# Routed rows of an eight-expert layer: transposed on TensorE through the identity, or on VectorE in blocks of 32 by 32

## The chip, the cores and the metric

The kernel runs on one core of one Trainium2 chip. The metric is the time of one execution on the device in microseconds (us), from the first instruction to the end. Three runs of the kernel before are shown, and beside them one profiled execution, whose trace is read here. Engines are named as in the profile: PE is TensorE's matmul, PEld its load of weights, DVE is VectorE, ACT is ScalarE, POOL is GpSimd, SP is SyncE; a "q" behind a name (SPq) is the engine's sequencer, where DMAs are issued.

## What is computed

Attention in a window of 64 over 4 x 8 heads of 576 x 64 gives 2304 tokens of 512 features; a gated layer (512 to 1536 and back) follows, and then a layer of eight experts, of which each token takes the two with the highest noisy logits:

```python
logits = x @ w_gate
noise_scale = np.log1p(np.exp(x @ w_noise))
noisy_logits = logits + noise_scale * noise
top2 = np.argpartition(-noisy_logits, 2, axis=1)[:, :2]
...
for e in range(E):
    for k in range(2):
        mask = top2[:, k] == e
        h = np.maximum(x[mask] @ w1[e], 0.0)
        out[mask] += top2_w[mask, k, None] * (h @ w2[e])
```

All of it is in float32. The change touches only how x[mask] comes to TensorE.

## The kernel before

**Stages.** Attention fills about the first 100 us. The gated layer runs over six chunks of 384 tokens until some 574 us. While it runs, each chunk's tokens get their experts and their places, and POOL scatters their rows (2 KB each) with indirect DMAs into `routed_rows` in DRAM, sorted by expert. The last stage is the experts' work on 43 tiles of 128 rows, in order of expert; the end gathers each token's two rows of results from `expert_rows` in DRAM, scales and adds them, and writes `out`.

**One tile t of the experts' stage.** SP loads its 128 rows of 512 floats into one of two buffers of `x_row` (a row in each partition, one DMA, L510). TensorE wants the features in the partitions, so `pe_xT` transposes the rows with four matmuls against the identity into the PSUM bank `BANK_A` (L956). DVE (`dve_xT`) writes the high part of the bank to `xT_high` (L1641) and the rest to `xT_low` (L1643): a float32 product is made of three passes of rounded parts (`PRODUCTS`). `pe_up2` (L944) makes 24 matmuls of 512 columns into banks 0 and 1, `dve_relu` (L1664) writes `relu`, `pe_hT` (L985) makes eight transposes, `dve_hT` splits them into `hT_high` and `hT_low` (L1652, L1654), `pe_down2` (L972) makes 24 more matmuls into bank 5, `dve_y` (L1671) copies that to the one buffer `y_row`, and SP stores it (L514).

**The order on each engine is written by hand**, one tile interlaced with the next. PE's turn in steady state is hT(t-1), up2(t), xT(t+1), down2(t-1). DVE's is hT(t-1), relu(t), xT(t+1), y(t-1). SP's is the load of tile t+4, which waits until the buffer's rows have been transposed (`xT_done`), and then the store of tile t, which waits for y(t). Tiles 0 to 3 are interlaced with the last chunk's routing: its logits pass over PE and ACT to DVE, which picks the experts (`dve_top2`, `dve_slots`); POOL then scatters the chunk's rows; the load of tile 3 waits until these scatters have landed; `dve_table` and `dve_table_rows` make the table of the tiles.

**Beside it** ACT loads the weights of the expert after next in 16 pieces of 512 KB as soon as a slot is free, rounds them to a high part (L1256), and POOL subtracts that for the low part (L652). POOL's end works through the chunks: it waits until the tiles that a chunk needs are stored (a wait on `y_row_out` with a count from the table), issues the gathers (L668) and adds the rows that ACT has scaled (L681).

## Time and profile before

| | us |
|---|---|
| median of 3 runs | 1123.01 |
| lowest, highest | 1121.91, 1123.09 |
| the profiled execution | 1124.06 |
| its span, from the first to the last instruction | 1122.2 |
| mean granted clock of TensorE | 0.996 of 2.4 GHz |

The span is 1.9 us under the profiled execution's own time, which is 1.05 us over the median. In the views below a time at the start of a row is counted from the span's start. A busy share is a mean over stages with different limits; what an engine waited for stands in brackets behind a row of the timeline, and the end of the program is reached by following such waits back from the last instruction. A row of the timeline joins neighbouring instructions of one line (x2, x4).

### The profile page before, as it was taken

The numbers are of one execution on the slowest core, as the hardware profiler recorded it, in microseconds if no ns is written. First come the engines' busy times: TensorE is split into PE (matmuls) and PEld (weight loads), VectorE is DVE, ScalarE is ACT, GpSimd is POOL, SyncE is SP. The second block draws the span as 40 slices with busy tenths as digits, with TensorE's granted clock in tenths as the row PEclk, the third lists the DMA queues.
The fourth block names the chain that finished last, engine by engine and source line by source line (L and its number), as shares of the span: only waits on it lengthen the run. The fifth ranks groups of instructions, "written<-read, shape, count | busy, mean of one in ns | idle before, by whom it ended". The sixth has DMA issues, their size and how long they took to land.

```text
span 1122.2 us, 20144 instructions
## 1 busy us (share of the span) xinstructions
PE 1094.8 (98%) x6285; PEld 956.3 (85%) x6286; DVE 543.2 (48%) x1166; ACT 324.2 (29%) x712; POOL 398.5 (36%) x370
## 2 busy tenths in 40 slices
PE   8989999999999999999998999999999999999995
PEld 7878999999998999999986888888888888888884
DVE  6776344353353443353446744444544544454452
ACT  7996122332431431331462011110202020200331
POOL 3557992022022021100396033150707061421585
PEclk9999999999999999999999999999999999999998
DMA  7975527013022030000356133251516142311565
GB/s 213 274 239 186 166 83 272 1 57 113 1 92 80 1 134 18 39 19 1 123 187 233 41 104 131 65 171 43 196 37 195 45 157 77 118 62 54 184 219 180
DMA packets 82731, 129.39 MB, mean 115 GB/s; under 512 B 6592, under 2 KB 38736, under 8 KB 82672
## 3 DMA queue, kind: packets, MB, share of 16 engines
q1 hardware_dynamic: 60816, 71.20, 19.4%
q10 hardware_dynamic: 16032, 38.47, 10.6%
q0 software_dynamic: 5824, 18.95, 5.0%
q8 instruction: 34, 0.56, 0.2%
q14 instruction: 25, 0.20, 0.1%
HBM read 85.87 MB, written 42.73 MB: 115 GB/s over the span
## 4 chain that ended last, share of the span: by engine, by line
PE 86%; DMA 4%; POOL 3%; issue 3%; ACT 2%; DVE 1%; POOLq 0%; SPq 0%; ACTq 0%; DVEq 0%
PE bank L781 26%; PE bank L972 18%; PE bank L944 18%; PE bank L813 13%; PE bank L985 3%; PE bank L727 2%; PE bank L956 1%; PE bank L754 1%; PE bank L737 1%; POOL token_rows_a L668 1%; PE bank L721 1%; DMA token_rows_b<-expert_rows,slots_u 1%; ACT p_sb L1109 1%; PE bank L849 1%; POOL token_rows_a L681 1%
## 5 line engine op out<-in xcount | busy, mean ns | idle before, releaser
L781 PE MATMUL bank<-x_parts,mlp_weights 128*128 128x384 f32 x1704 | 312.0, 337 | 0.0
L781 PEld LDWEIGHTS bank<-x_parts,mlp_weights 128*128 128x128 f32 x1704 | 296.8, 188 | 5.9 <-issue 0.7
L972 PE MATMUL bank<-expert_parts,hT_high 128*128 (+1 forms) x688 | 216.1, 395 | 1.4 <-DVE hT_low L1654 1.4
L944 PE MATMUL bank<-expert_parts,xT_high 128*128 (+1 forms) x688 | 215.9, 395 | 0.5 <-DVE xT_low L1643 0.5
L652 POOL TENSOR_TENSOR expert_parts<-raw_expert_a,expert_parts 128x512 fp32r<-128x512 f32 x64 | 81.4, 1301 | 259.8 <-ACT expert_parts L1256 259.7
L813 PE MATMUL bank<-mlp_weights,hidden_parts 128*128 128x512 f32 x648 | 162.1, 394 | 1.8 <-ACT y_sb L1180 1.8
L972 PEld LDWEIGHTS bank<-expert_parts,hT_high 128*128 128x128 f32 x688 | 126.1, 188 | 26.1 <-issue 1.7
L944 PEld LDWEIGHTS bank<-expert_parts,xT_high 128*128 128x128 f32 x688 | 126.0, 188 | 24.7 <-DVE xT_low L1643 0.8
L813 PEld LDWEIGHTS bank<-mlp_weights,hidden_parts 128*128 128x128 f32 x648 | 120.1, 188 | 25.2 <-ACT y_sb L1180 2.2
L972 PE MATMUL bank<-expert_parts,hT_low 128*128 (+1 forms) x344 | 134.5, 391 | 0.0
L944 PE MATMUL bank<-expert_parts,xT_low 128*128 (+1 forms) x344 | 134.4, 391 | 0.0
L619 POOL DMA_INDIRECT routed_rows<-y_sb,slot_now x36 | 35.8, 994 | 261.4 <-DVE slot_now L1482 252.3
L1256 ACT CAST expert_parts<-raw_expert_a 128x1024 fp32r<-128x1024 f32 x32 | 33.6, 1050 | 303.7 <-PE bank L972 269.3
L1671 DVE COPY y_row<-bank 128x512 f32<-128x512 f32 x43 | 29.8, 692 | 158.7 <-PE bank L972 158.1
L1409 DVE TENSOR_TENSOR hidden<-bank,sigmoid 128x384 f32<-128x384 f32 x72 | 40.1, 557 | 135.3 <-ACT sigmoid L1161 129.2
L1664 DVE TENSOR_SCALAR relu<-bank 128x512 f32<-128x512 f32 x86 | 59.3, 691 | 94.5 <-PE bank L944 94.5
L1172 ACT CAST hidden_parts<-hidden 128x384 fp32r<-128x384 f32 x72 | 37.0, 513 | 161.0 <-DVE hidden L1412 154.1
L652 POOL TENSOR_TENSOR expert_parts<-raw_expert_b,expert_parts 128x512 fp32r<-128x512 f32 x64 | 81.0, 1295 | 0.0
L1161 ACT ACTIVATE sigmoid<-bank 128x384 f32<-128x384 f32 x72 | 35.4, 492 | 149.0 <-PE bank L781 148.8
L972 PEld LDWEIGHTS bank<-expert_parts,hT_low 128*128 128x128 f32 x344 | 64.6, 188 | 13.8
L944 PEld LDWEIGHTS bank<-expert_parts,xT_low 128*128 128x128 f32 x344 | 64.6, 188 | 13.6
L1415 DVE TENSOR_TENSOR hidden_parts<-hidden,hidden_parts 128x384 fp32r<-128x384 f32 x72 | 48.5, 673 | 47.0 <-ACT hidden_parts L1172 47.0
(205 smaller groups left out, 1239.0 us busy)
## 6 DMA issues: line engine op xcount, KB each, us to landing
raw_expert_a<-in_w ACTq DMA_DIRECT2D x32, 512.0 KB, 3.6
raw_expert_b<-in_w ACTq DMA_DIRECT2D x32, 512.0 KB, 4.1
x_row<-routed_rows SPq DMA_DIRECT2D x43, 256.0 KB, 2.7
expert_rows<-y_row SPq DMA_DIRECT2D x43, 256.0 KB, 2.0
expert_rows<-zeros SPq DMA_DIRECT2D x4, 2304.0 KB, 12.7
v_sb<-in_v SPq DMA_DIRECT2D x32, 256.0 KB, 3.6
q_sb<-in_qT SPq DMA_DIRECT2D x16, 288.0 KB, 3.6
k_sb<-in_kT SPq DMA_DIRECT2D x16, 288.0 KB, 4.0
```

The lines of the kernel that those rows point to most:

```text
L619: nc.gpsimd.indirect_dma_start(out=xs_dram, out_offset=bass.IndirectOffsetOnAxis(ap=slot_now[:, t, r:r + 1], axis=0), in_=y_sb[:, t, :], i ...
L652: nc.gpsimd.tensor_tensor(ew_sb[:, slot, 2 * kind + 1, at:at + 512], raw_exp(q)[:, half * 512:half * 512 + 512], ew_sb[:, slot, 2 * kind, ...
L781: last = nc.tensor.matmul(bank[:, 0:CHUNK], w_sb[:, i, wp, at:at + P], xp[:, par, part, k, :], start=n == 0, stop=n == 3 * KB - 1)
L813: last = nc.tensor.matmul(ps[3 + t][:, 0:D], hp[:, i % 2, part, t * P:(t + 1) * P], w_sb[:, i, wp, 2 * KB * P:COLS], start=i == 0 and n == ...
L944: last = nc.tensor.matmul(ps[half][:, 0:512], (xTh, xTl)[xp][:, k, :], ew_sb[:, bass.ds(slot, 1), wp, k * F2 + half * 512:k * F2 + half * ...
L972: last = nc.tensor.matmul(ps[5][:, 0:D], (hTh, hTl)[hp][:, f, :], ew_sb[:, bass.ds(slot, 1), 2 + wp, f * D:(f + 1) * D].rearrange("p a n - ...
L985: last = nc.tensor.transpose(ps[2 + b][:, f * P:(f + 1) * P], relu[:, col:col + P], ident[:])
L1161: nc.scalar.activation(sig[:], ps[2 * i % 3][:, 0:CHUNK], ACT.Sigmoid).then_inc(sig_done, 1)
L1172: nc.scalar.copy(hp[:, i % 2, 0], h_sb[:]).then_inc(hh_done, 1)
L1409: nc.vector.tensor_tensor(h_sb[:], ps[2 * i % 3][:, 0:CHUNK], sig[:], ALU.mult).then_inc(gated, 1)
L1415: nc.vector.tensor_tensor(hp[:, i % 2, 1], h_sb[:], hp[:, i % 2, 0].bitcast(F32), ALU.subtract).then_inc(hl_done, 1)
L1664: nc.vector.tensor_scalar(relu[:, half * 512:half * 512 + 512], ps[half][:], 0.0, None, ALU.max).then_inc(relu_done, 1)
```

## The change

The four matmuls against the identity are gone from PE, for every tile, and with them `pe_xT` and the argument `between` of `pe_down2`. DVE makes one instruction in their place, a transpose of [128, 512] floats in blocks of 32 by 32, each block inside its own 32 partitions, into a new buffer `x_transposed` in SBUF; the two instructions behind it that make the high and the low part now read this buffer and no longer a PSUM bank. A block must already lie in the quarter of the partitions in which it is to end, so the load of a tile becomes four DMAs, one for each quarter s: partition 32s + r gets, for k and q from 0 to 3, the 32 floats of row 32q + r that begin at column 128k + 32s. A quarter is 64 KB, in pieces of 128 bytes. The waits move with it: DVE waits for the rows (now 64 counts a tile) and for `xT_low` of the tile before, then transposes, and waits for `up_done` as before. The loop of DVE now runs over pairs of tiles, since the buffer's number has to be known. `is_e` and `of_e` lie at another address.

```diff
-                sp.dma_start(x_row[:, buf, :], xs_dram[bass.ds(row, P), :]).then_inc(x_row_in[buf], 16)
+                rows = xs_dram[bass.ds(row, P), :].rearrange("(q r) (k s c) -> s r k q c", r=BLOCK, s=BLOCKS, c=BLOCK)
+                for s in range(BLOCKS):
+                    sp.dma_start(x_row[s * BLOCK:(s + 1) * BLOCK, buf, :].rearrange(
+                        "r (k q c) -> r k q c", k=KB, c=BLOCK), rows[s]).then_inc(x_row_in[buf], 16)
...
-        def pe_xT(pe, t, buf, before):
-
-            pe.wait_ge(x_row_in[buf], 16 * before + 16)
-            if not (isinstance(t, int) and t == 0):
-                pe.wait_ge(xTl_done, t)
-            for k in range(KB):
-                last = nc.tensor.transpose(BANK_A[:, k * P:(k + 1) * P], x_row[:, buf, k * P:(k + 1) * P], ident[:])
-            last.then_inc(xT_done, 1)
...
-                if buf is not None:
-                    pe_xT(pe, t + 1, buf, earlier)
...
-        def dve_xT(dve, t):
+        def dve_xT(dve, t, buf, earlier):
+
+            dve.wait_ge(x_row_in[buf], 16 * BLOCKS * earlier + 16 * BLOCKS)
+            if not (isinstance(t, int) and t == 0):
+                dve.wait_ge(xTl_done, t)
+            nc.vector.transpose(x_T[:].rearrange("p k t -> p (k t)"), x_row[:, buf, :]).then_inc(xT_done, 1)
+            if not (isinstance(t, int) and t == 0):
+
+                dve.wait_ge(up_done, 2 * t)
             dve.wait_ge(xT_done, t + 1)
-            if not (isinstance(t, int) and t == 0):
-
-                dve.wait_ge(up_done, 2 * t)
-            bank = BANK_A[:].rearrange("p (k t) -> p k t", k=KB)
-            nc.vector.tensor_copy(xTh[:], bank).then_inc(xTh_done, 1)
+            nc.vector.tensor_copy(xTh[:], x_T[:]).then_inc(xTh_done, 1)
             dve.wait_ge(xTh_done, t + 1)
-            nc.vector.tensor_tensor(xTl[:], bank, xTh[:].bitcast(F32), ALU.subtract).then_inc(xTl_done, 1)
+            nc.vector.tensor_tensor(xTl[:], x_T[:], xTh[:].bitcast(F32), ALU.subtract).then_inc(xTl_done, 1)
```

On PE, in the loop over the tiles, where up2 of one tile ends and down2 of the tile before begins, this stands in a row before:

```order
L944 MATMUL bank<-expert_parts,xT_high 128x512
L944 MATMUL bank<-expert_parts,xT_low 128x512
L956 MATMUL bank<-ident,x_row 128x128 x4
L961 ISA
L972 ISA
L972 MATMUL bank<-expert_parts,hT_high 128x512
```

and this now (L953 is pe_up2's line in the changed file, L969 that of pe_down2):

```order
L953 MATMUL bank<-expert_parts,xT_high 128x512
L953 MATMUL bank<-expert_parts,xT_low 128x512
L960 ISA
L969 ISA
L969 MATMUL bank<-expert_parts,hT_high 128x512
```

The four transposes are gone and nothing has taken their place.

On DVE, in the same loop, from the second half of relu(t) to the copy of y(t-1), before:

```order
L1664 TENSOR_SCALAR relu<-bank 128x512
L1636 REGISTER_ALU
L1639 ISA
L1641 CAST xT_high<-bank 128x512
L1643 TENSOR_TENSOR xT_low<-bank,xT_high 128x512
L1670 ISA
L1671 COPY y_row<-bank 128x512
```

and now:

```order
L1661 TENSOR_SCALAR relu<-bank 128x512
L1630 ISA
L1632 REGISTER_ALU
L1633 STREAM_TRANSPOSE x_transposed<-x_row 128x512
L1636 REGISTER_ALU
L1637 REGISTER_ALU
L1638 CAST xT_high<-x_transposed 128x512
L1640 TENSOR_TENSOR xT_low<-x_transposed,xT_high 128x512
L1667 ISA
L1668 COPY y_row<-bank 128x512
```

One instruction came in ahead of the two that split, and these read SBUF.

On DVE at the start of the experts' stage, around tile 1, where the last chunk's logits pass through, before:

```order
L1664 TENSOR_SCALAR relu<-bank 128x512
L1430 COPY logitsT<-bank 96x128
L1641 CAST xT_high<-bank 128x512
L1643 TENSOR_TENSOR xT_low<-bank,xT_high 128x512
L1434 COPY logits<-bank 128x48
L1652 CAST hT_high<-bank 128x512
```

and now:

```order
L1661 TENSOR_SCALAR relu<-bank 128x512
L1423 COPY logitsT<-bank 96x128
L1633 STREAM_TRANSPOSE x_transposed<-x_row 128x512
L1638 CAST xT_high<-x_transposed 128x512
L1640 TENSOR_TENSOR xT_low<-x_transposed,xT_high 128x512
L1427 COPY logits<-bank 128x48
```

The new instruction stands ahead of the copy of the logits.

## Rows read from the trace of the kernel before

**Rows 1.** The page: busy time by engine, and the chain that ended last

```profile
PE 1094.8 (98%) x6285; PEld 956.3 (85%) x6286; DVE 543.2 (48%) x1166; ACT 324.2 (29%) x712; POOL 398.5 (36%) x370
...
PE 86%; DMA 4%; POOL 3%; issue 3%; ACT 2%; DVE 1%; POOLq 0%; SPq 0%; ACTq 0%; DVEq 0%
```

**Rows 2.** Windows: us, busy PE PEld DVE ACT POOL, clock, DMA share, GB/s

```profile
797.50:809.75 12.25, 12.25 (x62) 10.23 (x61) 5.94 (x10) 2.64 (x3) 8.89 (x8) 1.00 0.64 215
809.75:822.00 12.25, 12.25 (x62) 10.23 (x61) 5.94 (x9) 0.00 (x0) 0.00 (x0) 1.00 0.12 43
```

**Rows 3.** One line, L956: duration ns min/median/max, first and last start

```profile
L956 PE MATMUL bank<-ident,x_row x172: 270/273/329, 569.7 to 1085.7; 128*128 128x128 f32 x172
```

**Rows 4.** Timeline of PE, start and us, up2 to down2, transposes between

```profile
803.30 0.40 PE L944 MATMUL bank<-expert_parts,xT_low 128*128 x1
803.53 0.60 PE L956 MATMUL bank<-ident,x_row 128*128 128x128 f32 x4
...
804.44 0.40 PE L972 MATMUL bank<-expert_parts,hT_low 128*128 x1
```

**Rows 5.** Timeline of PE, tile 2, up2 to down2, nothing between

```profile
604.98 0.39 PE L944 MATMUL bank<-expert_parts,xT_low 128*128 128x512 f32 x1
...
605.20 0.62 PE L972 MATMUL bank<-expert_parts,hT_high 128*128 128x512 f32 x2
...
605.66 0.39 PE L972 MATMUL bank<-expert_parts,hT_low 128*128 128x512 f32 x1
```

**Rows 6.** Timeline of the same steady tile: DVE, and PE's next up2

```profile
803.74 0.69 DVE L1664 TENSOR_SCALAR relu<-bank 128x512 f32<-128x512 f32 x1 [1.95 <-PE bank L944]
...
804.34 0.68 DVE L1641 CAST xT_high<-bank 128x512 fp32r<-128x512 f32 x1
...
805.06 0.69 DVE L1643 TENSOR_TENSOR xT_low<-bank,xT_high 128x512 fp32r<-128x512 f32 x1
...
810.25 0.71 PE L944 MATMUL bank<-expert_parts,xT_high 128*128 x2
```

**Rows 7.** Single lines: a DVE operation with two SBUF inputs, POOL's subtraction

```profile
L1415 DVE TENSOR_TENSOR hidden_parts<-hidden,hidden_parts x72: 557/559/1724, 110.0 to 571.2; 128x384 fp32r<-128x384 f32 x72
...
L652 POOL TENSOR_TENSOR expert_parts<-raw_expert_a,expert_parts x64: 1272/1290/1612, 557.7 to 983.9; 128x512 fp32r<-128x512 f32 x64
```

**Rows 8.** DMA from 10 to 12 us, a DMA's issue, x_row's landing

```profile
DMA packets 1355, 0.58 MB, mean 289 GB/s; under 512 B 797, under 2 KB 1231, under 8 KB 1355
...
q1 hardware_dynamic: 1355, 0.58, 102.1%
...
122.22 0.51 SPq L452 DMA_DIRECT2D raw_mlp<-in_w_val  x1
...
DMA to landing us min/median/max: 2.5/2.7/6.6
```

**Rows 9.** Timeline, start of the experts' stage: waits of PE and POOL

```profile
584.35 0.73 PE L944 MATMUL bank<-expert_parts,xT_high 128*128 128x512 f32 x2 [0.52 <-DVE xT_low L1643]
...
594.24 0.97 POOL L619 DMA_INDIRECT routed_rows<-y_sb,slot_now  x1 [5.76 <-DVE slot_now L1482]
...
598.54 0.31 PE L893 MATMUL bank<-ident,table_columns 128*1 128x43 f32 x4 [0.79 <-DVE table_columns L1573]
...
605.48 1.45 SPq L510 DMA_DIRECT2D x_row<-routed_rows  x2
...
610.35 0.66 PE L956 MATMUL bank<-ident,x_row 128*128 128x128 f32 x4 [0.90 <-DMA x_row<-routed_rows]
...
614.16 0.71 PE L944 MATMUL bank<-expert_parts,xT_high 128*128 x2
```

**Rows 10.** The end: POOL's last wait for a store, last adds, y's copies

```profile
1058.50 0.95 POOL L668 DMA_INDIRECT token_rows_a<-expert_rows,slots_u  x1 [5.01 <-DMA expert_rows<-y_row]
...
1112.20 3.70 POOL L681 TENSOR_TENSOR token_rows_b<-token_rows_b,token_rows_a 128x512 f32<-128x512 f32 x3 [3.67 <-ACT token_rows_b L1298]
...
L1671 DVE COPY y_row<-bank x5: 692/692/693, 1067.1 to 1111.3; 128x512 f32<-128x512 f32 x5
```

More of the change, by code:

```diff
@@ L21 @@
 GROUP = 3
+BLOCK = 32
+BLOCKS = P // BLOCK
 def window_start(j):
@@ L158, in attention_moe_kernel @@
     yT_last = at("yT_last", [P, CHUNK_TILES, KB, P], F32, mlp.pos)
+    under = Area(mlp.pos)
+    is_e = under.take("is_e", [P, 2 * TILES, E], F32)
+    of_e = under.take("of_e", [P, 2 * TILES, E], F32)
     xc = mlp.take("x_chunk", [P, KB, CHUNK], F32)
@@ L190, in attention_moe_kernel @@
     xTl = moe.take("xT_low", [P, KB, P], F32R)
+    x_T = moe.take("x_transposed", [P, KB, P], F32)
     relu = moe.take("relu", [P, F2], F32)
@@ L211, in attention_moe_kernel @@
     kept = moe.take("kept", [P, 2, TILES], F32)
-    is_e = moe.take("is_e", [P, 2 * TILES, E], F32)
-    of_e = moe.take("of_e", [P, 2 * TILES, E], F32)
     of_last = moe.take("of_last", [P, CHUNKS, E], F32)
@@ L900, in pe_chunk @@
                     pe_up(pe, c, i, par)
-                if last and i == FB - 1:
-                    pe_xT(pe, 0, 0, 0)
                 if not first and i == 4:
@@ L948, in pe_up2, with pe_down2 @@
                 last.then_inc(up_done, 1)
[L950 to L959 removed]
+        def pe_down2(pe, t, slot, expert):
             pe.wait_ge(expert_low, 16 * expert + 16)
@@ L968, in pe_down2 @@
                     pe.wait_ge(hTl_done, 2 * t + 1 + f // 4)
-                if between and f == FB2 - 2:
-                    between()
                 for wp, hp in PRODUCTS:
@@ L1010, in pe_experts, with tile @@
             pe_up2(pe, 2, 0, 0)
-            pe_down2(pe, 1, 0, 0, lambda: pe_xT(pe, 3, 1, 1))
+            pe_down2(pe, 1, 0, 0)
             pe.wait_ge(table_done, 1)
-            def tile(t, buf, earlier=0):
+            def tile(t):
                 now = entry(pe, t + T_SLOT, 1), entry(pe, t + T_E, E - 1)
@@ L1019, in tile @@
                 pe_up2(pe, t, *now)
-                if buf is not None:
-                    pe_xT(pe, t + 1, buf, earlier)
                 pe_down2(pe, t - 1, *before)
                 return now
-            tile(3, 0, 2)
-            tile(4, 1, 2)
+            tile(3)
+            tile(4)
             with pe.Fori(0, (ETILES - 7) // 2) as m:
-                tile(2 * m + 5, 0, m + 3)
-                tile(2 * m + 6, 1, m + 3)
-            tile(ETILES - 2, (ETILES - 1) % 2, (ETILES - 1) // 2)
-            now = tile(ETILES - 1, None)
+                tile(2 * m + 5)
+                tile(2 * m + 6)
+            tile(ETILES - 2)
+            now = tile(ETILES - 1)
             pe_hT(pe, ETILES - 1)
@@ L1692, in dve_experts @@
             dve_relu(dve, 2)
-            dve_xT(dve, 3)
+            dve_xT(dve, 3, 1, 1)
             dve_y(dve, 1)
@@ L1697, in dve_experts, with tile @@
                 dve_relu(dve, t)
-                dve_xT(dve, t + 1)
+                dve_xT(dve, t + 1, (t + 1) % 2, (t + 1) // 2)
                 extra(dve, link)
                 dve_y(dve, t - 1)
-            with dve.Fori(5, ETILES - 1) as t:
+            def tile(t, buf, earlier):
                 dve_hT(dve, t - 1)
                 dve_relu(dve, t)
-                dve_xT(dve, t + 1)
+                dve_xT(dve, t + 1, buf, earlier)
                 dve_y(dve, t - 1)
+            with dve.Fori(0, (ETILES - 7) // 2) as m:
+                tile(2 * m + 5, 0, m + 3)
+                tile(2 * m + 6, 1, m + 3)
+            tile(ETILES - 2, (ETILES - 1) % 2, (ETILES - 1) // 2)
             t = ETILES - 1
```

11 lines of the change are left out of this document (4 added, 7 removed).

## The prediction

> **What bounds the kernel now.** I read the page first: PE is busy 98% of the span, and the chain that ended last runs over PE for 86% of it [rows 1]. The windows say what that means in the stage that changes: two neighbouring tiles take 12.25 us each with PE busy for all of it, one of them while an expert's weights arrive (POOL busy 8.89 us, DMA share 0.64), one with POOL idle (DMA share 0.12) [rows 2]. So in steady state a tile costs what PE's instructions cost, whatever stands beside it, and DVE is busy for 5.94 of 12.25 us. Then I read the two ends of the stage. At its start PE waits for others three times: 0.52 for xT_low of tile 1, 0.79 for the table, 0.90 for the rows of tile 3 [rows 9]. At its end the last thing that waits for a tile is POOL, at 1058.50, for a store of y; five copies of y follow it, the last at 1111.3, and nothing waits for them: the 43 tiles are numbered 0 to 42, so the store waited for is that of tile 37 [rows 10]. From there to the end of the span, 63.7 us, gathers and adds of POOL set the time (its last adds start at 1112.20, behind ACT and a gather). What PE gains after tile 37 is therefore worth nothing.
>
> **What leaves PE.** 172 transposes, four for each of 43 tiles [rows 3]. Each row says 273 ns, but PE's instructions overlap, so I take the pitch. With transposes, the third matmul of down2 starts 804.44 - 803.30 = 1.14 us after the last one of up2 [rows 4]; in tile 2, where nothing stands between, it starts 605.66 - 604.98 = 0.68 us after it [rows 5]. A tile's transposes cost 0.46 us. An upper bound is 0.60, the merged row of the four; a lower one, if the loads of weights behind them hide less than I think, 0.40.
>
> **How many count.** PE runs xT(t+1) ahead of down2(t-1), so ahead of y(37) stand the transposes up to tile 39. Tiles 0 to 4 belong to the start, which is worked out below. Tiles 5 to 39 are 35: 35 x 0.46 = 16.1 us, all on the path. Tiles 40 to 42 come too late.
>
> **What DVE gets.** One transpose of 128 x 512. No row has one. The nearest are the DVE operations of the same shape, 0.68 to 0.69 us [rows 6]; below, 0.35, if it ran at two elements a cycle; above, twice, 1.4. I take 0.69, since it moves as many elements. The cast and the subtraction now read SBUF; I take 0.68 and 0.69 for them as before. In the steady tile DVE ends its last relu and starts the cast at 804.34; the chain now is transpose, cast, subtraction at a pitch of 0.72 [rows 6], so xT_low is ready at about 806.5 and not at 805.75. PE wants it for the next up2 at 810.25 [rows 6], and 0.46 earlier with the change: 809.79. From 804.34 that leaves 5.45 us for a chain of 2.1. What hides the new instruction is down2 of the tile before; it is hidden until it takes 4.0 us. Behind it on DVE wait y(t-1) and hT, whose inputs come only with the end of down2, shortly ahead of that next up2. DVE's load rises to about 6.6 of 11.8 us. Cost: nothing.
>
> **POOL and DVE on SBUF.** The subtraction had one input in SBUF and now has two. The row of such an operation, at 384 columns, has a median of 559 ns and a maximum of 1724, and POOL's subtraction takes 1290 ns [rows 7]: an operation of DVE can lose about 1.2 us where POOL works. In a burst of weights the chain would then take up to 2.1 + 1.2 for the subtraction, and 1.2 more if the cast is hit as well, 4.5 us in all, still under 5.45. It is hidden in steady state; it counts at the start and at the end, where these chains lie open. The Trainium skill states the rule behind it (SBUF — State Buffer, Who interferes with whom): VectorE with two inputs in SBUF, or in a 2-port mode, and GpSimd exclude each other from a shared pair of ports for a whole instruction. The long maximum in [rows 7] fits it; by the rule a cast from SBUF would be struck too, which no row here shows.
>
> **The load.** One DMA becomes four, and 128 packets of 2 KB become 2048 of 128 bytes, 128 on each of 16 engines. From 10 to 12 us the queues were full and passed 1355 packets of 428 bytes on average, 797 of them under 512 bytes, in 2 us x 16 x 1.02 = 32.7 us of engines' time: 24 ns a packet [rows 8]. The small ones cost at most that; so a tile's load costs up to 128 x 24 = 3.1 us on each engine, where now it is some 0.7 (half of 0.12 x 12.25, [rows 2]). The share in a burst goes from 0.64 to at most 0.85: not full. In time: a row with a three-level pattern takes SP 0.51 us to issue [rows 8], so four take 2 us instead of 0.34, and the landing, 2.5 to 6.6 us [rows 8], grows by up to 2.4. The load of a tile is issued some 23 us ahead of its use (two tiles), so about 9 us are hidden with 14 to spare. Behind the loads on SP and in its queue waits the store of y, which has to land within a tile (11.8 us) since y_row is one buffer; SP issues the load behind the transpose, at about 805 in this tile, and the store only behind down2 and y's copy, after 809, so that is covered as well. The Trainium skill warns here (DMA: Bandwidth & Descriptors, Specifications): under 512 bytes a transfer leaves line rate, with a read-modify-write. By that rule alone the load might be several times dearer than by its bytes; the rows above already hold that price, and the sum is made from them.
>
> **The start.** Here DVE and the load are on the path. Tile 0: DVE comes to it out of the last chunk's work at the same time as before; the chain ends 0.7 later while PE comes 0.46 earlier; I count no gain. Tile 1: PE waits already 0.52 for xT_low, and the copy of the logits, on which experts, scatter and table hang, stands behind this chain [rows 9]. It gets 0.72 longer, and POOL is at work there: +0.5 to +3, I take +0.9. Tile 2: the same chain stands ahead of the table for which PE waits 0.79 [rows 9]: +0.7 more, but that delay ends in PE's later wait. Tile 3: its load is issued at 605.48 when the scatter has landed; the scatter began at 594.24 behind DVE's slots [rows 9], so it moves by the 0.9. From 606.4: the issue of the fourth piece 1.6 us later, landing after 4.9 as before (605.48 to 610.35) plus 0.5, so about 613.4; then DVE's chain of 2.1 and 0.7 for POOL: up2 of tile 3 at 616.2, and not at 614.16 [rows 9]. That is +2.0; behind it the transposes of tile 4 are gone, -0.46. The start costs **1.6 us**, with ends at 0 and 7 (every chain hit by POOL, the load at its slowest landing in a full queue).
>
> **The end.** POOL's chain of 63.7 us stays. Three tiles' chains on DVE meet it: 0 to 4 us; I take 0.5.
>
> **Sum.** 16.1 - 1.6 - 0.5 = 14.0 us less. The profiled execution would have a span of 1122.2 - 14.0 = 1108.2 and a time of 1110.1; the median stands 1.05 below it: **1109.0**. The bounds: 35 x 0.40 = 14.0, less 7 and less 1, and 35 x 0.60 = 21 with a start at 1: 1117 and 1103. That both ends of all terms meet is unlikely.
>
> **Rivals.**
> 1. POOL and DVE block each other more than I take. Speaks for it: the maximum of [rows 7]; against it: the median there. Each open chain then loses both waits: the start 3.5, the end 4: 16.1 - 7.5 = 8.6 less, **1114.4**. This is also where the rule of the Trainium skill on the shared ports leads.
> 2. The small packets are slow beside the weights' packets, not enough to bound a tile, but tile 3 and the store behind tile 4's load come late at the start, by 6 to 10 us (the queue is full there: the slowest landing, 6.6 us, was in this stretch). 16.1 - 10 = 6 less, **1117**.
> 3. Slower: DVE's transpose is dear. The mechanism is the chain from relu to xT_low ahead of the next up2; it decides from 4.0 us for the instruction. At 5.5, eight times the row of its shape, the chain would be 1.5 us too long: 35 x (1.5 - 0.46) = +36, **1161**. Against it: every operation of this shape takes 0.7.
> 4. Slower: the load bounds the tile. It decides from 11.8 us a load, 92 ns a packet. At 18 us, a tile costs 18 and not 12.25: 34 x 5.75 = +195, **1320**. Against it: the 24 ns of [rows 8].
> 5. The change does not do what it says: PE's gain is taken back by a wait that I do not see (a landing that comes only with the fourth quarter, hT late behind a blocked DVE), and the time stays: **1123**.
>
> **How the numbers follow.** The forecast has a chance of 0.66, rival 1 0.15, rival 2 0.08, rivals 3 and 4 0.07 together, rival 5 0.04. The range holds the forecast and rival 1: 1104 to 1115.5, 0.81. A measurement of this kernel can tell about 0.2% from no change, 2.2 us. Faster by more: 0.66 + 0.15 + 0.08 = 0.89; within: 0.04; slower: 0.07.
>
> **What would show it.** Right, if in the changed kernel's trace the steady tiles are 11.8 us apart with PE busy throughout, if the transpose takes 0.7 us, if PE's wait ahead of up2 of tile 3 is 1 to 3 us, and if POOL still waits last for the store of tile 37, at about 1044, with the end 64 us behind. Wrong, if PE waits for xT_low or hT_low in steady tiles, if the loads land later than 12 us after their issue, if DVE or POOL operations of 1.5 us and more are frequent on the open chains, or if after the last wait for a store POOL's chain has grown.

## The result and the profile after

| | before | after |
|---|---|---|
| median of 4 runs, us | 1122.53 | 1110.66 |
| lowest, highest | 1121.91, 1123.09 | 1109.55, 1111.26 |
| ratio, 95% interval | | 0.9893 (0.9876 to 0.991) |
| the profiled execution | 1124.06 | 1109.55 |
| its span | 1122.2 | 1107.7 |

The forecast was 1109.0, in a range from 1104 to 1115.5, with a span of 1108.2. The page of the changed kernel begins and goes on thus (engines with busy time, share and instructions, a queue with its packets, the chain that ended last; before: [rows 1]):

```profile
PE 1076.5 (97%) x6113; PEld 940.3 (85%) x6114; DVE 587.5 (53%) x1209; ACT 324.2 (29%) x712; POOL 404.6 (37%) x370
...
q1 hardware_dynamic: 145440, 71.20, 22.9%
...
PE 87%; POOL 4%; issue 3%; DMA 2%; DVE 2%; ACT 1%; SPq 0%; POOLq 0%; ACTq 0%; DVEq 0%
```

PE has 172 instructions fewer and is 18.3 us less busy, DVE has 43 more and is 44.3 us more busy. PE still carries the chain. Two neighbouring tiles of the steady state, windows with the columns of [rows 2], the second one beside an expert's weights:

```profile
833.20:845.00 11.80, 11.80 (x58) 9.86 (x57) 6.39 (x10) 2.45 (x3) 3.60 (x3) 1.00 0.36 89
845.00:856.78 11.78, 11.78 (x57) 9.82 (x56) 8.30 (x10) 4.93 (x5) 11.78 (x10) 1.00 0.82 233
```

PE is busy for every microsecond of both, so a tile costs 11.79 where it cost 12.25. DVE's three instructions per tile, grouped over all 43 tiles (ns min/median/max):

```profile
L1633 DVE STREAM_TRANSPOSE x_transposed<-x_row x43: 697/701/712, 570.8 to 1071.2; 128x512 f32<-128x512 f32 x43
...
L1638 DVE CAST xT_high<-x_transposed x43: 426/428/1511, 571.5 to 1072.0; 128x512 fp32r<-128x512 f32 x43
L1640 DVE TENSOR_TENSOR xT_low<-x_transposed,xT_high x43: 691/693/1672, 572.4 to 1072.4; 128x512 fp32r<-128x512 f32 x43
```

The start of the stage, the timeline of PE, DVE and POOL (in brackets the wait before a row):

```profile
585.88 0.73 PE L953 MATMUL bank<-expert_parts,xT_high 128*128 128x512 f32 x2 [2.11 <-DVE xT_low L1640]
...
594.21 0.97 POOL L630 DMA_INDIRECT routed_rows<-y_sb,slot_now  x1 [5.99 <-DVE slot_now L1475]
...
612.00 0.71 DVE L1633 STREAM_TRANSPOSE x_transposed<-x_row 128x512 f32<-128x512 f32 x1 [5.42 <-DMA x_row<-routed_rows]
612.82 1.51 DVE L1638 CAST xT_high<-x_transposed 128x512 fp32r<-128x512 f32 x1
614.37 0.69 DVE L1640 TENSOR_TENSOR xT_low<-x_transposed,xT_high 128x512 fp32r<-128x512 f32 x1
...
615.41 1.21 PE L953 MATMUL bank<-expert_parts,xT_high 128*128 x2 [3.25 <-DVE xT_low L1640]
```

And the window from 612 to 620 us; its clock of 0.79 is a mixture of TensorE's two levels, 2.4 and 1.2 GHz, and PE had stood idle for 3.25 us before its row at 615.41:

```profile
612.00:620.00 8.00, 4.75 (x16) 3.72 (x15) 5.16 (x7) 0.00 (x0) 2.04 (x2) 0.79 0.77 212
```

The end, from the timeline of POOL and from the chain that ended last (start, us, what):

```profile
1045.66 0.95 POOL L679 DMA_INDIRECT token_rows_a<-expert_rows,slots_u  x1 [4.65 <-DMA expert_rows<-y_row]
```

```profile
1040.73 0.70 DVE y_row L1668
1041.60 3.30 DMA expert_rows<-y_row
...
1081.83 4.09 DMA token_rows_b<-expert_rows,slots_u
```

**Where the 14.5 us of span are.** I cut both traces at the same four events. In the last column stands what the prediction's terms say for the piece.

| piece | before | after | difference | forecast |
|---|---|---|---|---|
| first up2 to the copy of y(0) | 24.12 | 24.78 | +0.66 | |
| y(0) to y(4) | 52.06 | 52.77 | +0.71 | see below |
| y(4) to y(37), 33 tiles | 404.36 | 389.06 | -15.30 | -0.46 a tile |
| y(37) to POOL's last wait for a store | 3.68 | 4.93 | +1.25 | 0 |
| from there to the end | 63.7 | 62.0 | -1.66 | +0.5 |

The five pieces add to -14.3, and the first up2 itself came 0.16 us earlier: -14.5 in all. (Of 35 tiles' transposes, two fall into the first two pieces. The copy of y(37) came 14.1 us earlier; against 35 x 0.463 = 16.2 the start therefore lost 2.1, where the forecast had 1.6.)

### The profile page after: what moved, and what is told of

It is laid out like the page before. It is cut to its first block, busy times and chain, and to the rows that moved or that the text cites. A ratio compares the mean times of both kernels' runs of the same rounds, so it can differ in the third digit from the quotient of the medians.

```text
span 1107.7 us, 20151 instructions
## 1 busy us (share of the span) xinstructions
PE 1076.5 (97%) x6113; PEld 940.3 (85%) x6114; DVE 587.5 (53%) x1209; ACT 324.2 (29%) x712; POOL 404.6 (37%) x370
## 4 chain that ended last, share of the span: by engine, by line
PE 87%; POOL 4%; issue 3%; DMA 2%; DVE 2%; ACT 1%; SPq 0%; POOLq 0%; ACTq 0%; DVEq 0%
PE bank L792 26%; PE bank L953 18%; PE bank L969 18%; PE bank L824 13%; PE bank L982 3%; PE bank L738 3%; PE bank L765 2%; POOL token_rows_a L679 1%; PE bank L748 1%; PE bank L732 1%; PE bank L860 1%; DMA token_rows_b<-expert_rows,slots_u 1%; POOL token_rows_a L692 1%; ACT p_sb L1102 1%; PE bank L871 1%
## 5 line engine op out<-in xcount | busy, mean ns | idle before, releaser
L953 PE MATMUL bank<-expert_parts,xT_high 128*128 (+1 forms) x688 | 217.2, 397 | 6.2 <-DVE xT_low L1640 5.4
L969 PE MATMUL bank<-expert_parts,hT_high 128*128 (+1 forms) x688 | 212.0, 389 | 1.5 <-DVE hT_low L1651 1.5
L953 PEld LDWEIGHTS bank<-expert_parts,xT_high 128*128 128x128 f32 x688 | 126.6, 189 | 31.4 <-issue 4.7
L969 PEld LDWEIGHTS bank<-expert_parts,hT_high 128*128 128x128 f32 x688 | 129.0, 188 | 28.3 <-issue 1.7
L953 PE MATMUL bank<-expert_parts,xT_low 128*128 (+1 forms) x344 | 134.8, 392 | 0.0
L969 PE MATMUL bank<-expert_parts,hT_low 128*128 (+1 forms) x344 | 134.1, 390 | 0.0
L663 POOL TENSOR_TENSOR expert_parts<-raw_expert_b,expert_parts 128x512 fp32r<-128x512 f32 x64 | 86.3, 1381 | 0.6 <-ACT expert_parts L1249 0.6
L953 PEld LDWEIGHTS bank<-expert_parts,xT_low 128*128 128x128 f32 x344 | 64.8, 188 | 14.0
L969 PEld LDWEIGHTS bank<-expert_parts,hT_low 128*128 128x128 f32 x344 | 64.6, 188 | 13.4
```

Source lines behind the costliest of these rows:

```text
L663: nc.gpsimd.tensor_tensor(ew_sb[:, slot, 2 * kind + 1, at:at + 512], raw_exp(q)[:, half * 512:half * 512 + 512], ew_sb[:, slot, 2 * kind, ...
L953: last = nc.tensor.matmul(ps[half][:, 0:512], (xTh, xTl)[xp][:, k, :], ew_sb[:, bass.ds(slot, 1), wp, k * F2 + half * 512:k * F2 + half * ...
L969: last = nc.tensor.matmul(ps[5][:, 0:D], (hTh, hTl)[hp][:, f, :], ew_sb[:, bass.ds(slot, 1), 2 + wp, f * D:(f + 1) * D].rearrange("p a n - ...
```

## Experiments

The profile left two theories on the start open. **The load**: the rows come late because of the four DMAs with 128-byte pieces. **DVE and POOL**: the three operations on SBUF are held beside POOL's subtractions. A third suspect is TensorE's clock after a wait. All kernels were timed against the kernel before on the same chip; the runs lie on four chips, and before had medians of 1121.19 (the first four runs below), 1122.48 (the next four), 1124.04 (the three with PSUM) and 1123.0 (the last). The stages ahead end at slightly different moments (the first up2 between 571.9 and 577.4 us), so I compare distances:

| kernel | ratio (95%) | first up2 to y(0) | y(0) to y(4) |
|---|---|---|---|
| before | 1 | 24.12 | 52.06 |
| changed, first profile | 0.9893 (0.9876, 0.991) | 24.78 | 52.77 |
| changed, again | 0.9918 (0.9905, 0.9931) | 26.12 | 53.03 |
| plain load | 0.9906 (0.9891, 0.9922) | 26.10 | 53.13 |
| blocked load, PE transposes | 1.005 (1.0032, 1.0068) | 23.37 | 57.25 |
| PE for tiles 0 to 3 | 0.9859 (0.9839, 0.9878) | 23.38 | 49.79 |
| filled wait | 0.9894 (0.9869, 0.9918) | 26.15 | 51.44 |
| transpose into PSUM | 0.987 (0.9853, 0.9886) | 25.29 | 51.96 |
| plain load, into PSUM | 0.9827 (0.9811, 0.9844) | 24.39 | 48.06 |
| PE for tile 3 alone, others into PSUM | 0.9858 (0.9841, 0.9875) | 24.87 | 48.76 |

**1. The changed kernel again**, as the measure for the runs beside it.

> The changed kernel once more, beside the three runs that take parts of it, on their chip. Theory (A): the gain is 0.46 us a tile for tiles 5 to 39, less what the start of the experts' stage loses (about 2.3 us until down2 of tile 2, by the first profile). Expected: 11 to 13 us faster than before, ratio 0.989, y's copies 11.78 us apart, PE's wait ahead of up2 of tile 3 near 3.2 us. Rival (B): part of what was seen was the luck of one profile (the end 1.7 us shorter, a store 1.3 us later); then these two places differ in this profile while the time stays.

Median 1112.12 (1111.59 to 1112.36, 6 runs). It lost more of the start than the first profile: the clock was 0.93 from 575 to 600 us (first profile: 1.00) and the first up2 to y(0) took 1.3 us more. So the fall of the clock behind the first wait, 2.1 us long in both, comes in some executions or on some chips and not in others. Its price went on: the scatter began 21.41 us after the first up2, in the first profile 20.09.

**2. The plain load with DVE's transpose.**

```diff
-                rows = xs_dram[bass.ds(row, P), :].rearrange("(q r) (k s c) -> s r k q c", r=BLOCK, s=BLOCKS, c=BLOCK)
-                for s in range(BLOCKS):
-                    sp.dma_start(x_row[s * BLOCK:(s + 1) * BLOCK, buf, :].rearrange(
-                        "r (k q c) -> r k q c", k=KB, c=BLOCK), rows[s]).then_inc(x_row_in[buf], 16)
+                sp.dma_start(x_row[:, buf, :], xs_dram[bass.ds(row, P), :]).then_inc(x_row_in[buf], 16)
```

> The changed kernel with one plain DMA of 2 KB rows a tile in place of the four in pieces of 128 bytes; DVE's transpose stays. The rows are then laid out wrongly, so the experts work on permuted values, in the same shapes and with the same routing. Theory (A), the load costs only at tile 3, where it is waited for: rows there 1.5 us earlier, PE's wait ahead of up2 of tile 3 about 1.7 us and not 3.2, steady tiles still 11.78 apart; 1.5 to 3 us faster than the changed kernel. Rival (B), the small packets also slow weights, stores or gathers all along: steady tiles or the end get shorter as well, and it is 4 us or more faster. Rival (C), the start's loss is DVE's chain alone: no change.

1111.23 (1109.72 to 1111.58, 5 runs), 0.9 us under the changed kernel on the same chip; PE's wait ahead of up2(3) is still 3.34. Read at that point, it seemed that the load costs nothing. The timeline of DVE and POOL says otherwise:

```profile
609.85 0.71 DVE L1630 STREAM_TRANSPOSE x_transposed<-x_row 128x512 f32<-128x512 f32 x1 [0.34 <-DMA x_row<-routed_rows]
610.67 6.61 DVE L1635 CAST xT_high<-x_transposed 128x512 fp32r<-128x512 f32 x1
617.31 0.69 DVE L1637 TENSOR_TENSOR xT_low<-x_transposed,xT_high 128x512 fp32r<-128x512 f32 x1
```

```profile
607.02 5.03 POOL L660 TENSOR_TENSOR expert_parts<-raw_expert_a,expert_parts 128x512 fp32r<-128x512 f32 x4
612.01 4.97 POOL L660 TENSOR_TENSOR expert_parts<-raw_expert_b,expert_parts 128x512 fp32r<-128x512 f32 x4
```

The rows stand 4.4 us earlier than in the run before it (609.85 against 614.25), and then a cast of 0.43 us takes 6.61: it ends at 617.28, just after POOL's run of subtractions, which ends at 616.98. In the repeated changed kernel the cast ended at 616.65 behind a POOL that ended at 616.37, in the first profile at 614.33 behind 614.04. In these two, though, no more than the last two subtractions of POOL's run were left. So in run 2 the end of POOL's run, and not the landing, set the moment. Runs 9 and 10 test what the load would save if the cast were not held.

**3. The blocked load alone**, with TensorE's transposes as before.

```diff
-            pe.wait_ge(x_row_in[buf], 16 * before + 16)
+            pe.wait_ge(x_row_in[buf], 16 * BLOCKS * before + 16 * BLOCKS)
```

(and the four DMAs of the change.)

> The kernel before with the load in four parts of 128-byte pieces, and TensorE's transposes kept; the rows are laid out wrongly here too, so the experts work on permuted values. Theory (A): the load alone costs 1.5 to 3 us at tile 3 (landing later, store of y behind it) and nothing else: 1123.5 to 1126 us, steady tiles 12.25 apart. Rival (B), the packets hurt all along: over 1128 us. Rival (C): no change at all, 1122.5.

1128.01 (1122.15 to 1131.13, 9 runs): 5.6 us slower than before by the ratio, with an interval from 3.6 to 7.6. Steady tiles stay 12.25 us apart. What its profiled execution (1130.03) lost between the first up2 and the end lies at tile 3: y(0) to y(4) is 5.2 us longer. PE's wait there, and the window around it:

```profile
614.82 1.12 PE L962 MATMUL bank<-ident,x_row 128*128 128x128 f32 x4 [4.60 <-DMA x_row<-routed_rows]
```

```profile
612.00:620.00 8.00, 5.18 (x19) 4.46 (x20) 2.62 (x4) 0.00 (x0) 2.81 (x3) 0.60 0.81 216
```

The wait was 0.90 before [rows 9], so 3.7 are the load's. The rest I put down to the clock: four transposes take 1.12 where they took 0.66. In the steady state the load is free, as forecast; at the start it is not. Theory (A) had the place right and the size too low (1.5 to 3 us).

**4. TensorE transposes tiles 0 to 3 (with plain loads), DVE the rest.**

```diff
+                if isinstance(t, int) and t < 4:
+                    sp.dma_start(x_row[:, buf, :], xs_dram[bass.ds(row, P), :]).then_inc(x_row_in[buf], 16)
+                    return
...
+            pe_xT(pe, 2, 0, 1)
             pe_down2(pe, 0, 0, 0)
```

> Tiles 0 to 3 as before (plain load, transposes on TensorE, split out of PSUM), tiles 4 to 42 as in the changed kernel. Theory (A): the open chains at the start are then those of before, up2 of tile 3 starts near 614.2, the full clock holds there, and 35 or 36 x 0.46 remain: about 2.3 to 2.7 us faster than the changed kernel, near 1108 us, ratio to before 0.987. Rival (B): the loss moves to tile 4, whose blocked load is issued at the same place, and the store of y behind it: less than 1 us faster than the changed kernel.

1104.56 (1103.51 to 1106.96, 4 runs): 7.6 us under the changed kernel on the same chip, three times what I had expected. Both pieces of the start are shorter than those of the changed kernel, by 2.7 and 3.2 us, the clock is 1.00 in all windows of the start, and PE waits 0.52 at up2(1), as before the change, and not at all at up2(3). That is 6.0 us; another 1.9 is that its first up2 came earlier, at 573.18 and not at 575.11, and that is 1.1 earlier than in the kernel before (574.28), which does the same work up to there; so I count it as the execution's. The costs of the start add up: a wait, the clock behind it, the later store.

**5. The wait ahead of up2(3) filled** with 28 transposes of the identity.

```diff
+                if isinstance(t, int) and t == 3:
+                    fill(28, BANK_A)
                 pe_up2(pe, t, *now)
```

> The changed kernel with 28 transposes of the identity, into a bank that nothing reads, between hT(2) and up2 of tile 3, where PE idled 3.25 us and its clock then read 0.79 of full over 612 to 620 us. Theory (A): the idle time lowers the granted clock, and up2 of tile 3 took 6.9 us and not 5.6 for that; filled, the clock stays at 1.00 and up2(3) takes 5.6: 1.3 us faster than the changed kernel. Rival (B): the slow matmuls come from something else (the port contention, late weights): they stay slow, and the time is unchanged.

1111.36 (1109.0 to 1113.22, 4 runs). PE's window from 612 to 620 us:

```profile
612.00:620.00 8.00, 7.81 (x54) 6.91 (x53) 3.28 (x3) 1.26 (x2) 5.96 (x5) 1.00 0.99 284
```

The same window of the repeated changed kernel:

```profile
612.00:620.00 8.00, 4.76 (x23) 3.77 (x22) 5.05 (x7) 1.06 (x1) 4.37 (x4) 0.91 0.98 267
```

The clock stays at 1.00 where it was 0.91, and from 620 to 632 us it is 1.00 where it was 0.92. In both kernels up2(3) begins 16.5 us after the copy of y(0), so its operands came no sooner, and yet y(0) to y(4) takes 51.44 and not 53.03. So the idle time is what brings the clock down, and the clock alone is worth 1.6 us there. The medians do not settle it: the two ratios differ by 0.0024, and their intervals overlap.

**6 and 7. DVE's work lengthened**, by three and by six more transposes a tile from tile 6 on, each waiting for the last.

```diff
+            if not (isinstance(t, int) and t < 6):
+                for i in range(3):
+                    nc.vector.transpose(x_T[:].rearrange("p k t -> p (k t)"), x_row[:, buf, :]).then_inc(more, 1)
+                    dve.wait_ge(more, 3 * t + (i + 1 - 6 * 3))
```

> The changed kernel with three more DVE transposes (same data, same target) ahead of the one of each tile from tile 6 on: 2.3 us more on the chain from relu to xT_low. Theory (A): the chain has 3.5 us of cover behind down2 (xT_low ready at 660.4, up2 at 663.9 in the changed kernel's trace), so steady tiles stay 11.78 us apart and the time stays within 1 us. Rival (B): DVE is nearer to being the bound than its waits say (hT behind y, or GpSimd's port): tiles get longer, up to 34 x 2.3 = 78 us.

> The same with six more, 4.6 us. Theory (A): that is 1.1 us beyond the cover; tiles from 6 on are 12.8 to 13.0 us apart and PE waits for xT_low about 1.1 us in each; 34 tiles make +37 to +42 us on the changed kernel, 1148 to 1152 us, somewhat more if PE's clock falls in the waits. Rival (B): the cover is given by hT, not by xT_low: then PE's waits stand ahead of down2 instead. Rival (C): the cover is larger, and nothing changes.

Three more: 1119.27 (1116.63 to 1132.97, 10 runs), ratio 0.9985 (0.9956, 1.0014). I had expected it within 1 us of the changed kernel; that failed: against before it is 0.15% faster, where the repeated changed kernel was 0.82%, so about 7.5 us are lost. Most tiles stay 11.8 us apart, but two behind tile 4 take 12.2 and 12.7, and every tenth or so takes 13.04, where the chain stands beside POOL (5.1 us between y(4) and y(37)). Another 2.8 us come behind y(37); 1.1 of them because SP issues its store, behind four loads, 2.0 us after the copy began and not 0.9. A tile in which the chain meets POOL:

```profile
732.60 2.19 DVE L1636 STREAM_TRANSPOSE x_transposed<-x_row 128x512 f32<-128x512 f32 x3
734.83 0.71 DVE L1638 STREAM_TRANSPOSE x_transposed<-x_row 128x512 f32<-128x512 f32 x1
735.57 1.60 DVE L1643 CAST xT_high<-x_transposed 128x512 fp32r<-128x512 f32 x1
737.21 1.65 DVE L1645 TENSOR_TENSOR xT_low<-x_transposed,xT_high 128x512 fp32r<-128x512 f32 x1
```

```profile
739.20 0.72 PE L954 MATMUL bank<-expert_parts,xT_high 128*128 x2 [0.93 <-DVE xT_low L1645]
```

From 732.60 to 738.86 are 6.26 us, and PE waits 0.93: the cover is 5.3 us, where the prediction had 5.45. The transposes themselves keep their 0.71 us beside POOL; cast and subtraction are held by 1.2 and 1.0.

Six more: 1177.9 (1176.31 to 1184.65, 6 runs), ratio 1.0489 (1.0467, 1.051). A quiet tile takes 13.09, 1.3 us too long. Seven transposes, cast and subtraction take about 6.4 us, 1.0 more than the cover, and PE waits that long ahead of up2; what adds the other 0.3 is open. I had expected 1148 to 1152; the rest comes from tiles of 14.4 to 15 us in each burst of weights, from one of 20.8, in which the cast was held for as long as POOL worked, and from the clock (mean 0.97 between 660 and 1020 us):

```profile
951.63 8.11 DVE L1643 CAST xT_high<-x_transposed 128x512 fp32r<-128x512 f32 x1
```

```profile
949.58 4.98 POOL L664 TENSOR_TENSOR expert_parts<-raw_expert_a,expert_parts 128x512 fp32r<-128x512 f32 x4
954.53 4.92 POOL L664 TENSOR_TENSOR expert_parts<-raw_expert_b,expert_parts 128x512 fp32r<-128x512 f32 x4
```

That is the exception. In the same run five casts met runs of POOL's subtractions at nearly the same point, 0.80 to 0.84 us into one of them, and took 0.72 to 0.77; the one above began 0.78 us into one. One of the five:

```profile
679.85 0.77 DVE L1643 CAST xT_high<-x_transposed 128x512 fp32r<-128x512 f32 x1
```

**8. PE's work put back in one place**: 48 transposes of the identity between up2(4) and down2(3).

```diff
                 pe_up2(pe, t, *now)
+                if isinstance(t, int) and t == 4:
+                    fill(48, BANK_A)
```

> The changed kernel with 48 transposes of the identity (5.1 us of TensorE) between up2(4) and down2(3). Theory (A): before tile 37 PE sets the end, so all of it shows: +5.1 us, 1115.8. Rival (B): PE's time there is covered by DVE, which had extra work in tiles 3 and 4: less than 3 us show.

1115.95 (1115.54 to 1119.61, 4 runs), ratio 0.994 (0.9921, 0.9959), as expected. y(0) to y(4) is 58.39, 5.36 more than in the repeated changed kernel. The next 33 tiles took 389.08 us, as in the changed kernel (389.06), so none of it is won back. What PE gains ahead of tile 37 counts in full.

**9. DVE's transpose into a PSUM bank.** The cast and the subtraction then have no more than one input in SBUF.

```diff
-            nc.vector.transpose(x_T[:].rearrange("p k t -> p (k t)"), x_row[:, buf, :]).then_inc(xT_done, 1)
+            xT = BANK_A[:].rearrange("p (k t) -> p k t", k=KB)
+            nc.vector.transpose(BANK_A[:], x_row[:, buf, :]).then_inc(xT_done, 1)
...
-            nc.vector.tensor_copy(xTh[:], x_T[:]).then_inc(xTh_done, 1)
+            nc.vector.tensor_copy(xTh[:], xT).then_inc(xTh_done, 1)
...
-            nc.vector.tensor_tensor(xTl[:], x_T[:], xTh[:].bitcast(F32), ALU.subtract).then_inc(xTl_done, 1)
+            nc.vector.tensor_tensor(xTl[:], xT, xTh[:].bitcast(F32), ALU.subtract).then_inc(xTl_done, 1)
```

> The changed kernel, but VectorE's transpose writes a PSUM bank, from which the cast and the subtraction read; nothing else is different, and the result is the same. Theory A: beside GpSimd's weight subtractions an SBUF-only cast or subtraction of VectorE is held up (in the changed kernel's repeated run: cast 0.78 and subtraction 1.66 us at tile 0, 0.92 and 1.63 at tile 1, cast 1.59 at tile 3, and with the plain load one cast of 6.61 us), and reading PSUM takes that away. Then every cast takes 0.68 and every subtraction 0.69, nowhere more; the operands stand 0.9 us earlier at tile 3 and 1.2 us earlier at tile 1, TensorE's wait there falls from 3.25 to about 2.3 and from 2.1 to about 0.9, and the time is 2 to 3 us under the changed kernel's: 1109 to 1110 with before at 1121.5. Theory B, the long casts are late for another reason (a wait that the trace doesn't show) and PSUM only costs 0.25 us a tile: the long ones stay, and the time is 1112 to 1113.

1109.41 (1108.1 to 1109.71, 4 runs). The expectation took before at 1121.5; it was 1124.04 on this chip, so by the ratio, 0.987, the gain is 2 to 3 us more than expected. All casts and subtractions, in one view:

```profile
L1639 DVE CAST xT_high<-bank x43: 691/692/693, 570.3 to 1069.4; 128x512 fp32r<-128x512 f32 x43
L1641 DVE TENSOR_TENSOR xT_low<-bank,xT_high x43: 691/691/692, 571.1 to 1070.1; 128x512 fp32r<-128x512 f32 x43
```

Not one of 86 is long; in the changed kernel 13 of 43 casts and 14 of 43 subtractions took over 1 us. The theory of the SBUF port stands, the other falls. PE waits 0.97 at up2(1) (2.1) and 1.88 at up2(3) (3.25). The trace puts the second down to a subtraction of POOL that ended at 612.14, but the low part was ready at 611.94 and up2(3) began 0.36 behind that, at the same distance as in the changed kernel (615.06 and 615.41), and in run 10 up2(3) ran ahead of POOL's end; so I take it for the low part. y(0) to y(4) is 1.1 us shorter than in the repeated changed kernel, although the clock still fell behind the wait of 1.88 us:

```profile
612.00:620.00 8.00, 7.70 (x27) 6.21 (x28) 4.18 (x7) 0.00 (x0) 0.14 (x1) 0.79 0.51 146
```

The first piece gained nothing that lasts: PE now waits 1.35 for `so_far` and 1.95 for the table (1.44 in the repeated changed kernel), so the routing on DVE is what holds there.

**10. Both: the plain load of run 2 and the PSUM bank of run 9.**

> As the one before, but with a single plain load in place of the four blocked ones, so that the rows arrive 4.4 us earlier at tile 3 and the blocks stand in the wrong quarters (the products are not the reference's; the work is the same). With SBUF the plain load won 0.9 us only, since the cast of tile 3 then took 6.61 us, up to the end of GpSimd's run of subtractions. Theory A, that this was the shared SBUF port: the cast takes 0.68, the operands of tile 3 stand at about 612 us, before TensorE wants them at 614.5, the wait of 3.3 us and the fall of TensorE's clock after it are gone, and the time is 1106 to 1108 with before at 1121.5. Theory B: 1110 to 1112, as the plain load into SBUF.

1104.36 (1103.79 to 1105.69, 4 runs), ratio 0.9827, with before again at 1124.04. At tile 3 the rows stand at 606.12 and the chain is through before PE comes:

```profile
606.12 0.73 DVE L1631 STREAM_TRANSPOSE bank<-x_row 128x512 f32<-128x512 f32 x1 [0.48 <-DMA x_row<-routed_rows]
606.95 0.69 DVE L1636 CAST xT_high<-bank 128x512 fp32r<-128x512 f32 x1
607.68 0.69 DVE L1638 TENSOR_TENSOR xT_low<-bank,xT_high 128x512 fp32r<-128x512 f32 x1
```

There is no wait ahead of up2(3), and the clock stays:

```profile
612.00:620.00 8.00, 8.00 (x37) 6.64 (x36) 5.46 (x11) 0.00 (x0) 0.94 (x1) 1.00 0.29 95
```

With 1, 2 and 9 this makes a square of y(0) to y(4), its two rows from different chips: in SBUF 53.03 with the blocked and 53.13 with the plain load, in PSUM 51.96 and 48.06. The load costs nothing while the cast is held and 3.9 us once it isn't; the port costs 1.1 with the late rows and 5.1 with the early ones. In both large numbers the fall of the clock is contained. Each hid the other, and the first reading of run 2, that the load costs nothing, was wrong: a cost shown as zero beside another wait is only hidden.

**11. TensorE transposes tile 3 alone, PSUM for the others.**

```diff
-            pe_down2(pe, 1, 0, 0)
+            pe_down2(pe, 1, 0, 0, lambda: pe_xT(pe, 3, 1, 1))
```

(and the plain load for tile 3, and for all other tiles the PSUM bank of run 9.)

> The changed kernel with the transposes of tile 3 alone back on TensorE (from a plain load), placed before the last two blocks of down2(1), and VectorE's transpose into PSUM for all other tiles; the result is the same. The version with TensorE's transposes in tiles 0 to 3 gave a ratio of 0.9859. If the start's loss is at tile 3 (late rows, the held cast, the clock), this gives as much as that one: a ratio of 0.985 to 0.9875, 1104.5 to 1107 with before at 1121.5, the first value if TensorE's 3 x 0.46 us of transposes in tiles 0 to 2 come off the path, the last if VectorE's chain of 2.1 us at tile 1 makes TensorE wait 0.9 us there. If the loss sits in tiles 0 to 2 as well (the scatter delayed), it is 1108 or more.

1108.04 (1105.72 to 1109.52, 4 runs), a ratio of 0.9858, as expected and the same as run 4's 0.9859; the two were timed on different chips. y(0) to y(4) takes 48.76. Both pieces of the start together are within 0.5 us of run 4's. So TensorE's transposes need to come back at tile 3 alone. What the PSUM bank adds at tiles 0 to 2 is in this number too and was not taken apart; against run 9 (0.987) the ratio alone shows no gain.

**12. PE's work put at tile 41**, the 48 transposes of run 8.

```diff
                 pe_up2(pe, t, *now)
+                if isinstance(t, int) and t == ETILES - 2:
+                    fill(48, BANK_A)
```

> The changed kernel with 48 further 128x128 transposes of the identity on TensorE (5.1 us by the 0.107 us a piece of the run that had them at tile 4), placed between up2(41) and down2(40); the result is the same. The reading of the traces: what TensorE gains or loses after the copy of y(37) is worth nothing, since the last wait of GpSimd for a store is the one for y(37), and what follows is GpSimd's chain of gathers. Then y(37) stands where it did, only the copies y(40) to y(42) come 5 us later (the last at about 1101 to 1103.5), the end stays: 1110 to 1113 with before at 1121 to 1124, a ratio of 0.989 to 0.992. The rival, that TensorE's own end carries the end of the kernel: plus 5 us, 1115.5 to 1118, a ratio of about 0.994 to 0.996, as the same work at tile 4 gave.

1114.39 (1112.18 to 1115.44, 4 runs), ratio 0.9924 (0.9904, 0.9945): between the two forecasts, so that the times decide nothing. In its profiled execution (the lowest of the four) the added work is not in the chain: the copy of y(41) comes 5.2 us late (16.96 after the one ahead of it and not 11.8), the last one at 1101.02, the span ends at 1110.4. What is in the chain are three pieces, here in order of time:

```profile
1037.58 4.98 another core or an unknown queue
1042.68 0.70 DVE y_row L1674
...
1082.88 5.72 DMA token_rows_b<-expert_rows,slots_u
```

The copy of y(37) started 2.3 us after PE's down2(37) had ended (its next instruction is at 1040.33), and the gather of the last but one chunk landed in 5.72 us and not in 4.09. The same late copies of y(36) to y(38), 12.4 to 13.0 us apart with PE's tiles still 11.8, stand in the traces of runs 9 to 11; they are in none of runs 1 to 8. There y(37) came 1.4 to 2.1 us late, so those three kernels might be up to 2 us faster than they were. SP's issues of the loads were long at the same moments (4.67 us for four, not 2.93). Since the kernels have in common only the chip or the execution, and the changed code is not alike, I don't put it down to the edits, but that is not shown; what DVE waited for, the trace does not name. That PE's time behind y(37) is worth nothing thus rests on the chain of one profiled execution and not on the times.

## Why the prediction was right, and where it was not

**A tile, 0.46 us**: right. 33 tiles gave 15.30 us, 0.463 each.

**The transpose, 0.69**: 0.70. **The cast at 0.68**: it took 0.43 from SBUF, where POOL was quiet, and 0.69 from PSUM (run 9). By the Trainium skill (VectorE: DVE Perf Modes, Mode 2×_2P) a copy with its one source in SBUF may read it through both read ports, two elements a cycle, in float32 too; the shorter row fits that. It was of no use, since the chain was covered anyway, and it is the cast from SBUF that POOL can hold (run 2), while none from PSUM was held.

**The cover, 4.0 us for the instruction in 5.45**: 5.3 by run 6, so with the same two operations behind it an instruction of 3.9, and less beside POOL, where these two take 3.3 us and not 1.2.

**POOL and DVE**: the mechanism was right and the size was not. I took 0.7 us for tile 3 and bounded a held operation by 1.2. In the steady state that was so: 1.36 for the cast and 1.67 for the subtraction at 848 us, 3.8 us for the chain, hidden. The row at 848 us stands in the middle of a run of POOL's subtractions, and the cast was let in behind one of them, while the run became longer (5.68 us for four):

```profile
846.41 5.68 POOL L663 TENSOR_TENSOR expert_parts<-raw_expert_b,expert_parts 128x512 fp32r<-128x512 f32 x4
...
847.88 1.36 DVE L1638 CAST xT_high<-x_transposed 128x512 fp32r<-128x512 f32 x1
849.27 1.67 DVE L1640 TENSOR_TENSOR xT_low<-x_transposed,xT_high 128x512 fp32r<-128x512 f32 x1
```

But a cast that meets such a run can also be held to the end of all of it: 6.61 us in run 2 and 8.11 in run 7, while POOL's groups kept their 4.9 to 5.0. By the Trainium skill (SBUF — State Buffer, Who interferes with whom) whoever issues first gets the shared pair of ports for the whole instruction, and the other is blocked. The usual row agrees with that; the two long ones go beyond it, since the cast was blocked for five and for six whole instructions of 1.25 us in a row. What decides between the two cases stays open. That the changed kernel lost only 1.1 us at tile 3 was luck: the rows landed when POOL was nearly through, and run 2 shows what could have come. One sign that the prediction had named against itself did show: of the eight casts and subtractions of tiles 0 to 3, three took 1.5 us or more (1.66, 1.63, 1.51). The time held even so, since at tile 1 ACT's delay covered it in the first profile. Rival 1, which took both waits for every open chain, was not what happened: the waits do not add where the routing holds anyway.

**The load in steady state**: right. Between 616 and 628 us queue q1 passed 3631 packets, mostly of 128 bytes, in 32.0% of 16 engines x 12 us = 61 us, 17 ns a packet with one store among them; 24 was the bound. The share of a tile in a burst was 0.82 (bound 0.85). The issue is dearer than I took:

```profile
L520 SPq DMA_DIRECT2D x_row<-routed_rows x172: 582/582/1332, 562.4 to 1051.5; - x172
...
DMA to landing us min/median/max: 2.2/2.6/5.4
```

Four take 2.9 us with what lies between, not 2.0.

**The start, 1.6**: 2.1. The +0.9 at tile 1 was a wrong step for the first profile. PE's wait there grew from 0.52 to 2.11, but the scatter began 20.09 us after the first up2 and before the change 19.96: before, ACT came to the logits only 2.3 us after DVE had copied them, and that covered the longer chain. Where the clock fell behind this wait, the scatter did move: it began at 21.41 in the repeated run, and on the same chip at 19.21 in runs 3 and 4, which keep TensorE's transposes there. That the wait lowers the clock is what the step lacked. Tile 3 took the opposite way: up2(3) began at 615.41, 1.25 late and not 2.0, but then came two things that are not in the sum, TensorE's clock at 0.79 and the store of y(0), issued at 611.92 behind the eight loads of tiles 3 and 4 (before: at 606.98, behind two), for which y(1) waited 2.66 us. The forecast of 1.6 was near by errors of both signs. In the repeated run the clock fell in two stretches, and the start cost more.

**The end, +0.5**: -0.4. POOL's last wait for a store is for tile 37, as read; it ended at 1045.66, forecast about 1044. The piece from y(37) to that wait, taken as unchanged, grew by 1.25: its store took 3.30 us. The piece was 3.67 with the plain load (run 2) and 4.3 to 5.0 in runs 1, 4, 5 and 8, so the blocked loads are the suspect; but run 3 has them too, with 3.67, and nothing here takes it further. The chain behind it was 1.66 shorter, 1.5 of it in a gather that landed in 4.09 and not in 5.59 us. Both are landings, and run 12 shows the same gather at 5.72, so a difference of 1 us in this term says little.

**The sum**: a span 0.5 under the forecast, a median 1.7 over it. The profiled execution of before was 1.05 over its median, the one of after 1.1 under it; I had carried the first offset over to the changed kernel.

## What to carry to other kernels

A transpose taken from a saturated TensorE gives its pitch back in full, 0.46 us of a tile here, as long as the engine that takes it over has cover; do it where the work is hidden and leave the few open tiles as they were, which was worth some 6 us more than doing it everywhere (run 4). If GpSimd works in long runs, let VectorE's inputs on an open chain stand in PSUM: a cast from SBUF can be held until the run ends, though most were held for one instruction. And where one suspect costs nothing by itself, undo both before acquitting it.

## What the runs showed of the hardware

- A cast of 128x512 floats from SBUF took 0.43 us, from PSUM 0.68 to 0.69, and from SBUF beside GpSimd's back-to-back subtractions 0.7 to 1.9 as a rule, 6.61 and 8.11 in one case each (runs 2 and 7), and 3.5 and 4.4 beside its adds at the end of run 7; the 32 by 32 transpose of VectorE kept 0.70 to 0.71 us beside them, into SBUF, and 0.71 to 0.73 into PSUM.
- TensorE's clock, mean from 612 to 620 us: 0.79 around a wait of 3.25 us (first profile), 0.79 behind one of 1.88 (run 9), 0.60 around one of 4.60 (run 3), and 1.00 with the wait filled by small matmuls (run 5). With a wait of 2.1 us at tile 1 the mean from 575 to 600 us was 1.00 in the first profile and 0.93 in the repeated one.
- DMA pieces of 128 bytes took about 17 ns of a DMA engine's time each; SP needed 0.58 us for a DMA with this pattern.
- VectorE's copies of y started 1 to 3 us late beside the gathers in the traces of runs 9 to 12, behind something that the trace does not name. This stays open.
